# Ten stretches of discarded matmuls after the last output copies of a two-layer MoE kernel

## What is computed

```
w   = softmax over 7 taps of weight_gen              (8 heads)
x1  = sum_k w[..., k] * x[token - 6 + k]             per head of 24 features
y1  = (silu(x1 @ w_gate) * (x1 @ w_val)) @ w1_out    192 -> 1536 -> 192
h   = y1 @ w2_in                                     192 -> 2048
out = (h * clip(h + 3, 0, 6) / 6) @ w2_out           2048 -> 192
```

## Time and profile before

| | us |
|---|---|
| median of 2 runs | 1184.45 (1183.73 to 1185.17) |
| the profiled execution | 1184.21 |
| its span | 1182.4 |
| PE busy | 1175.9 (99%), 10379 matmuls |
| PEld busy | 1045.1 (88%) |
| DVE, ACT, POOL busy | 872.6, 635.3, 43.3 |
| mean granted TensorE clock | 1.000 |

### The profile page before, as it was taken

The page is one execution under the profiler, slowest core; times in us unless marked ns, Lnnn a source line. Parts: engine busy times, 40 slices in busy tenths (PEclk is TensorE's granted clock), DMA queues, the critical chain, the costliest instruction groups (busy, mean ns, idle before and its releaser), DMA issues.

```text
span 1182.4 us, 26082 instructions
## 1 busy us (share of the span) xinstructions
PE 1175.9 (99%) x10379; PEld 1045.1 (88%) x10379; DVE 872.6 (74%) x1335; ACT 635.3 (54%) x1107; POOL 43.3 (4%) x41
## 2 busy tenths in 40 slices
PE   8999999999999999999999999999999999999998
PEld 7898988898888989989899988988888899898887
DVE  7798777867778686786867769677696776864565
ACT  6657556364554645546455463654636546364564
POOL 6330000000000000000000000000000000000000
PEclk9999999999999999999999999999999999999999
DMA  7312020110202002020020300203002030100000
GB/s 227 104 42 66 1 79 1 40 40 3 76 1 61 19 7 74 1 62 19 9 70 1 79 1 11 69 1 79 1 14 65 1 79 1 20 26 3 13 7 21
DMA packets 78008, 44.28 MB, mean 37 GB/s; under 512 B 54364, under 2 KB 70236, under 8 KB 77784
## 3 DMA queue, kind: packets, MB, share of 16 engines
q1 hardware_dynamic: 77648, 42.48, 13.5%
q10 hardware_dynamic: 264, 0.34, 0.1%
HBM read 30.99 MB, written 11.80 MB: 36 GB/s over the span
## 4 chain that ended last, share of the span: by engine, by line
PE 98%; DMA 0%; SPq 0%; DVE 0%; ACT 0%; issue 0%
PE up_pair L1077 36%; PE acc L1092 25%; PE up_pair L1083 18%; PE acc L1099 16%; DMA stage<-in_moe_w_gate_dram 0%; PE acc L1388 0%; PE acc L1389 0%; PE acc L1395 0%; PE acc L1390 0%; PE acc L1396 0%; PE acc L1077 0%; PE acc L1083 0%; DVE in_tail_lo L909 0%; ACT in_tail_hi L598 0%; SPq L417 0%
## 5 line engine op out<-in xcount | busy, mean ns | idle before, releaser
L1077 PE MATMUL up_pair<-in_hi,up_hi 64*128 64x512 f32 x1268 | 349.5, 388 | 1.4 <-DVE hidden L890 0.7
L1077 PE MATMUL up_pair<-in_lo,up_hi 64*128 64x512 f32 x1268 | 348.5, 387 | 0.0
L1077 PE MATMUL up_pair<-in_hi,up_lo 64*128 64x512 f32 x1268 | 348.4, 387 | 0.0
L1092 PE MATMUL acc<-hid_lo,dn_hi 64*128 64x512 f32 x862 | 333.3, 387 | 0.0
L1092 PE MATMUL acc<-hid_hi,dn_lo 64*128 64x512 f32 x862 | 333.1, 386 | 0.0
L1099 PE MATMUL acc<-hid_lo,dn_tail 64*128 64x512 f32 x862 | 333.1, 386 | 0.0
L1092 PE MATMUL acc<-hid_hi,dn_hi 64*128 64x512 f32 x862 | 333.1, 386 | 0.0
L1099 PE MATMUL acc<-hid_hi,dn_tail 64*128 64x512 f32 x862 | 333.1, 386 | 0.0
L893 DVE SCALAR_TENSOR_TENSOR hidden<-hidden,up_pair 128x512 f32<-128x512 f32 x250 | 171.8, 688 | 183.3 <-ACT hidden L578 183.1
L898 DVE TENSOR_TENSOR hid_lo<-hidden,hid_hi 128x512 fp32r<-128x512 f32 x439 | 303.2, 691 | 2.3 <-ACT hid_hi L585 1.5
L578 ACT ACTIVATE hidden<-up_pair,half_col 128x512 f32<-128x512 f32 x250 | 172.0, 688 | 209.1 <-DVE hid_lo L898 147.4
(11 more groups left out here) (163 smaller groups left out, 1430.4 us busy)
## 6 DMA issues: line engine op xcount, KB each, us to landing
window<-in_x_dram SPq DMA_DIRECT2D x14, 960.0 KB, 5.3
out_dram<-out_rows SPq DMA_DIRECT2D x360, 16.0 KB, 1.5
turned_dram<-in_turned SPq DMA_DIRECT2D x56, 96.0 KB, 4.6
out_main<-turned_dram SPq DMA_DIRECT2D x14, 256.0 KB, 2.8
in_tail<-turned_dram SPq DMA_DIRECT2D x28, 128.0 KB, 3.0
stage<-in_moe_w_out_dram SPq DMA_DIRECT2D x7, 384.0 KB, 3.5
taps<-in_weight_gen_dram SPq DMA_DIRECT2D x1, 1568.0 KB, 7.0
stage<-in_moe_w_in_dram SPq DMA_DIRECT2D x4, 256.0 KB, 4.4
```

Source lines behind the costliest of these rows:

```text
L1077: return nc.tensor.matmul(dst[:, :], w[lane[half], col:col + P], a[lane[half], :], start=first and product == 0, stop=False)
L1092: return nc.tensor.matmul(acc[y][0], w[lane[half], k, :], a[lane[half], n % RING, :], start=half == LOW and product == 0 and k == 0, stop= ...
```

## The change

After `transpose_last()` TensorE waits for the two copies of the output rows, and then runs 528 matmuls whose products go to `up_bank` and are read by nobody. Their operands are `dn_hi[2]` (stationary, its first `width` columns) and the hidden tiles (moving, 512 columns), all written long before. A round in `lanes_of` is one matmul in each lane, a round in `quarters` one in each quarter of 32 rows, each into a bank of its own; a round in `whole` is one matmul of 128 rows. There are ten stretches of 24 rounds. Nothing else is changed.

```diff
             last_period(BLOCKS)
             transpose_last()
+            pe.wait_ge(s_far_rows, 1)
+            pe.wait_ge(s_near_rows, 1)
+            streams = [a[:, r, :] for r in range(RING) for a in (hid_hi, hid_lo)]
+            quarter = [slice(32 * q, 32 * q + 32) for q in range(4)]
+
+            def one(bank, rows, width, k, stream, start, stop):
+                nc.tensor.matmul(up_bank[bank][0:width, :], dn_hi[2][rows, k % N2, 0:width],
+                                 streams[stream % len(streams)][rows, :], start=start, stop=stop)
+
+            def lanes_of(rounds, low_width, high_width, bank=0):
+                for r in range(rounds):
+                    for half, width in ((LOW, low_width), (HIGH, high_width)):
+                        one(bank + half, lane[half], width, r, 2 * r + half, r == 0, r == rounds - 1)
+
+            def whole(rounds, width):
+                for r in range(rounds):
+                    one(0, slice(0, P), width, r, r, r == 0, r == rounds - 1)
+
+            def quarters(rounds, width):
+                for r in range(rounds):
+                    for q in range(4):
+                        one(q, quarter[q], width, r, r + q, r == 0, r == rounds - 1)
+
+            lanes_of(24, P, P)
+            lanes_of(24, 96, 96)
+            lanes_of(24, 64, 64)
+            lanes_of(24, 32, 32)
+            lanes_of(24, P, 64)
+            lanes_of(24, 64, P)
+            whole(24, P)
+            whole(24, 64)
+            quarters(24, P)
+            quarters(24, 64)
```

## The result

| | before | after |
|---|---|---|
| median, us | 1184.45 (1183.73 to 1185.17) | 1237.76 (1237.55 to 1237.98) |
| profiled execution, us | 1184.21 | 1237.55 |
| its span, us | 1182.4 | 1235.7 |
| mean granted clock | 1.000 | 1.000 |

A forecast was written before the change was run, and what follows sets the result against it. TensorE's matmul stream bounds the kernel (busy 99%). Start 1179.65 plus 54.88 for 240 rounds, first gap and layouts, 0.39 last matmul and the ending gave span 1235.2; 1.8 outside it made 1237.0 us, range 1234 to 1241.

The forecast's parts named there:

- When it starts: Hand-over from ScalarE: first added matmul 0.05 us after the s_far_rows copy ends at 1179.60, so at 1179.65.
- A round costs its moving columns, not its matmuls: Added stretches: tiles of a round run side by side, 0.227 us a round for 512 moving columns, 5.45 per 24 rounds.
- Loads are hidden: Added weight loads run beneath matmuls, also on the whole array; uncovered there they would add 0.11 each, 5.3 us in all.
- Narrower operands cost the same: Stretches with 96, 64 or 32 stationary columns: 0.227 us a round taken, floor 0.213; 0.235 throughout would add 1.9.
- Quarters of 32 rows: The last two stretches: four tiles side by side at 0.227 us a round, with no trace row; ceiling 0.91.
- Rival A: Quarter stretches: quarters don't run four abreast; 1247 or 1248 us in its cheap forms, 1270 without overlap; chance 0.11.
- Changes of layout: Lanes to whole array and whole array to quarters: 0.21 us extra each, 0.42 for two.
- Rival C: Mixed 64/128 stretches: each change of width is a change of layout, +9.9 us each, 1257; chance 0.03.
- The clock: Added part: the full 2.4 GHz is kept, with PE back after under half a microsecond; otherwise 0.43 us a round.
- rival B: Narrow stretches: the clock falls with few columns in use; 1242 us for 32 columns alone, 1266 for all six; chance 0.05.
- A slow restart after the gap: Start of the added work: a half-pace stretch as long as 2.85 us would add about 1.4 us.
- rival D: Program end: not slower, added matmuls free if done within 2.5 us of cover, about 11 rounds; 1184 us; chance 0.02.

The follow-up runs named there:

- Experiment 1: Changed kernel with its ten stretches replaced by fourteen of 24 rounds, first with 256 moving columns, then with 128: 1217.78 us.
- experiment 4: Changed kernel with all matmuls of a round on the same rows (0 to 63 for lanes, 0 to 31 for quarters), still into different banks: 1336.42 us.
- experiment 6: Changed kernel with the ten stretches replaced by three of 24 pairs of single rounds, a change of layout before each of 144 rounds: 1243.89 us.
- experiment 3: Changed kernel with only the first tile's matmul kept in each round of lanes and quarters, 240 matmuls instead of 528: 1271.72 us.
- experiment 7: Changed kernel with five stretches of 96 rounds instead: 32 wide in lanes, whole array, quarters and one single quarter, then lanes 128 wide: 1310.06 us.
- experiment 8: Changed kernel with one tile at a time instead, 128 wide: whole array, rows 0 to 63, rows 0 to 31, 0 to 63, whole, 0 to 63: 1298.67 us.
- experiment 9: Changed kernel with upper lane 32 wide, quarters 0 and 3, and quarter 3 alone instead, each after 24 whole-array rounds, then whole array: 1260.80 us.
- experiment 10: The unaltered kernel of experiment 3, timed again in several runs: 1242.71, 1242.85, 1270.91 and 1271.22 us.
- experiment 5: Changed kernel with TensorE also waiting for the last stores before the ten stretches, idle 2.9 us in place of 0.5: 1243.05 us.
- experiment 2: Changed kernel with only the first 8 rounds of the first stretch kept: 1183.97 us against 1183.81 for the kernel before, ratio 1.000.

## Why the prediction was right, point by point

- *When it starts.* 0.05 after the copy, as forecast; the copy itself was 0.08 later.
- *A round costs its moving columns, not its matmuls.* Shown by the ten stretches and by experiments 1 and 4: halving the columns halves the round, and taking the rows' difference away makes every matmul cost a round.
- *Loads are hidden.* On the whole array too: 5.57 us for that stretch, where an uncovered load each would have made it 8.1. Experiment 1 shows where they bind: a load of 128 columns sets the pace of a stream of 128; beside a stream of 256 a round with it took 6 ns more than one with a narrower operand.
- *Narrower operands cost the same.* Nearly: 96 and 64 wide took 0.230 a round and 32 wide 0.232, where I took 0.227 (5.53, 5.51 and 5.57 over 24). The mixed stretches took 0.231. All are inside the bound of 0.235, and together they make 0.4 of the 0.5 us by which the measured span exceeds the forecast one.
- *Quarters of 32 rows.* The one term without a row came out at the lanes' price. Rival A is refuted: 5.58 us with 96 matmuls.
- *Changes of layout.* 0.21 each was forecast from one sample; 0.23 and 0.22 in the kernel, 0.21 in experiment 6.
- *Changes of width.* Rival C is refuted: 11.07 us for the two mixed stretches. "TensorEngine Tiling (Array Packing)" of the Trainium skill (Key Properties) says that a change of tiling mode drains the engine; the changes between 128, 64 and 32 rows agree (0.21 each), a change of stationary width within lanes does not count as one here.
- *The clock.* It held, as forecast, and rival B is refuted in the form in which I put it, by columns. The fall itself exists, in other work: the stretches of 32 rows alone lost the full clock in experiments 3, 4, 7, 8, 9 and 10. The changed kernel streams through all 128 rows in every round, so it never met this. A slow restart after the gap was a risk that I priced at 1.4 us. With all rows in use and a longer gap it cost 2.9 (experiment 5). Where half of the rows were in use after the short gap, the clock fell in some executions, and that cost 28 (experiment 10); the fall came behind the gap, and its cause is open.
- *The end.* The barrier waits for TensorE: experiment 2 shows the other side of rival D's point, 8 rounds for nothing.
- *The sum.* 1235.2 for the span, 1235.7 measured; 1.8 outside it, 1.85 measured. TensorE's drain ended with its last matmul (1235.49), so the 0.05 added for it was not paid.

## What to carry to other kernels

Count rounds of tiles that run side by side, not matmuls: fewer stationary columns or fewer rows save nothing, and filling the other rows costs nothing. Keep the load shorter than the stream, since a longer one sets the pace. Add 0.2 us for each change of the row layout, and look at what ends last before pricing work at the end of a program, since some 2 us of it were free here. Before thinning out matmuls, look at the granted clock: leaving out three of a round's four tiles made it 1.9 times as long, some microseconds into the stretch.

## What the runs showed of the hardware

- Granted clock by what TensorE did: all 128 rows streaming, in one, two or four tiles and 32 to 128 columns wide, 1.00 throughout the added stretches, and back at 1.00 3.7 to 6.1 us after such a stretch began at 0.50. Rows 0 to 63, rows 64 to 127, or two quarters alone: 1.00 after work at 1.00, for up to 66 us, but for experiment 3, where it fell 2.2 us after rows 0 to 63 began. Rows 0 to 63 once it had fallen: 0.50, for up to 58 us; the others were not tried there. One quarter alone: fallen to 0.50 3.0 to 5.9 us after it began, in each of six stretches, and not back while it lasted.
- With these operands (float32r) a round at full clock takes 0.227 us for 512 moving columns, 0.113 to 0.120 for 256, and for 128 0.060, or 0.111 where the load is 128 wide. "TensorE: Matmul & The Clock Gate" of the Trainium skill (Wait — 56ns, not 53.3ns?) has N / 2.4 GHz plus a fixed 2.5 ns, which would be, by estimate, 0.216, 0.109 and 0.056; here the excess over the stream is 13 ns at 512 and, with narrow stationary operands, 7 at 256 and at 128.
- The two lanes of a mixed stretch (64 beside 128 wide) are 0.02 us apart at the end of it (1212.67 and 1212.69 above), and nothing is lost by it.
